# Turning the attention probabilities in squares of 32 on VectorE instead of on TensorE, in an attention + two-layer kernel in fp32

## What is computed

```python
# q, k, v: (4, 8, 576, 64), 2304 tokens of 512 values in all
mask = (rel >= 0) & (rel < 64)             # each query sees itself and 63 keys before it
attn = softmax(where(mask, q @ k.T / 8, -1e9))
x = (attn @ v)                             # as (2304, 512)
h = relu(x @ w_in);  x = (h * h) @ w_out   # first layer, 512 -> 2048 -> 512
h = x @ w_in2;  out = (h * cos(h)) @ w_out2   # second layer
```

## Time and profile before

| | us |
|---|---|
| median of 3 runs | 873.69 (873.03 to 874.81) |
| profiled execution | 873.09 |
| its span | 871.0 |
| TensorE busy in the span | 852.1 (98%), granted clock 1.0 |
| VectorE busy | 467.6 (54%) |
| ScalarE busy | 358.8 (41%) |
| GpSimd busy | 43.3 (5%) |

### The profile page before, as it was taken

One profiled execution on the slowest core, in us unless ns is written; L12 is line 12 of the kernel. 1 busy time (PEld: TensorE's weight loads), 2 busy tenths in 40 slices (PEclk: granted clock), 3 DMA queues, 4 the chain that ended last, 5 costly groups with the idle time before them and its releaser, 6 DMA issues.

```text
span 871.0 us, 13849 instructions
## 1 busy us (share of the span) xinstructions
PE 852.1 (98%) x5568; PEld 732.1 (84%) x5568; DVE 467.6 (54%) x805; ACT 358.8 (41%) x819; POOL 43.3 (5%) x51
## 2 busy tenths in 40 slices
PE   4899999999999999999999999999999999999998
PEld 4799988888888888888999888899999888888886
DVE  3776553335434453333556765666666565556554
ACT  4565443333333343323555433443444343334333
POOL 5500100000100000000000000000000000000000
PEclk9999999999999999999999999999999999999999
DMA  5645231111301130020331000300200200001001
GB/s 193 200 165 177 91 107 45 50 49 61 134 22 47 37 139 19 2 98 4 126 125 37 1 1 1 113 9 2 108 25 1 98 37 1 0 1 49 1 0 49
DMA packets 18928, 52.80 MB, mean 61 GB/s; under 512 B 2096, under 2 KB 2096, under 8 KB 17840
## 3 DMA queue, kind: packets, MB, share of 16 engines
q1 hardware_dynamic: 18864, 51.91, 17.3%
HBM read 41.42 MB, written 10.49 MB: 60 GB/s over the span
## 4 chain that ended last, share of the span: by engine, by line
PE 95%; DVE 2%; ACT 1%; DMA 1%; POOL 1%; issue 0%; SPq 0%; DVEq 0%; ACTq 0%
PE h L473 34%; PE y L515 23%; PE y L554 22%; PE st L473 11%; PE st L448 2%; PE st L417 2%; PE st L432 1%; DMA arena<-qk_duos 1%; PE y L417 1%; POOL arena L961 0%; ACT arena L625 0%; DVE arena L803 0%; DVE arena L793 0%; DVE w_out_lo L819 0%; PE h L448 0%
## 5 line engine op out<-in xcount | busy, mean ns | idle before, releaser
L824 DVE TENSOR_TENSOR act<-act 128x512 f32<-128x512 f32 (+1 forms) x80 | 51.1, 638 | 199.7 <-ACT g_hi L661 199.5
L655 ACT ACTIVATE act<-h 128x512 f32<-128x512 f32 (+1 forms) x80 | 44.4, 555 | 246.8 <-PE h L473 246.8
L832 DVE TENSOR_TENSOR g_lo<-act,g_hi 128x512 fp32r<-128x512 f32 (+1 forms) x160 | 102.5, 641 | 54.3 <-ACT g_hi L666 51.5
L515 PE MATMUL y<-g_hi,w_out_hi 128*128 128x512 f32 (+1 forms) x320 | 121.0, 378 | 1.0 <-DVE g_lo L832 1.0
L473 PE MATMUL h<-x_hi,w_in_hi 128*128 128x512 f32 (+3 forms) x488 | 120.7, 369 | 0.0
L473 PE MATMUL h<-x_hi,w_in_lo 128*128 128x512 f32 (+3 forms) x488 | 119.2, 365 | 0.0
L473 PE MATMUL h<-x_lo,w_in_hi 128*128 128x512 f32 (+3 forms) x488 | 118.8, 365 | 0.0
L515 PE MATMUL y<-g_lo,w_out_hi 128*128 128x512 f32 (+1 forms) x320 | 117.9, 369 | 0.0
L515 PE MATMUL y<-g_hi,w_out_lo 128*128 128x512 f32 (+1 forms) x320 | 117.7, 368 | 0.0
L554 PE MATMUL y<-w_out_hi,g_lo 128*128 128x512 f32 x288 | 112.7, 391 | 0.0
L554 PE MATMUL y<-w_out_lo,g_hi 128*128 128x512 f32 x288 | 112.6, 391 | 0.0
(11 more groups left out here) (81 smaller groups left out, 984.9 us busy)
## 6 DMA issues: line engine op xcount, KB each, us to landing
arena<-qk_duos SPq DMA_DIRECT2D x17, 640.0 KB, 4.4
arena<-w_in SPq DMA_DIRECT2D x32, 256.0 KB, 3.0
arena<-w_out SPq DMA_DIRECT2D x32, 256.0 KB, 2.8
arena<-v_duos SPq DMA_DIRECT2D x18, 384.0 KB, 3.5
out<-arena SPq DMA_DIRECT2D x18, 256.0 KB, 2.1
x_tiles<-x_hi SPq DMA_DIRECT2D x2, 1024.0 KB, 4.3
x_tiles<-x_lo SPq DMA_DIRECT2D x2, 1024.0 KB, 6.9
x_hi<-x_tiles SPq DMA_DIRECT2D x2, 1024.0 KB, 5.0
```

Source lines behind the costliest of these rows:

```text
L515: mm = pe.matmul(bank, w[:, f, d * P:(d + 1) * P], x[:, g % 2, c * size:(c + 1) * size], start=(s == 0 and c == 0 and n == 0 and d % per = ...
L655: nc.scalar.activation(act[:, g % 2, 0:cols1(g)], h_bank[g % 2][:, 0:cols1(g)], ACT.Relu).then_inc(relu_set, 1)
L824: nc.vector.tensor_tensor(a, a, a, ALU.mult).then_inc(sq_set, 1)
L832: nc.vector.tensor_tensor(g_lo[:, g % 2, cols], act[:, g % 2, cols], g_hi[:, g % 2, cols].bitcast(fp32), ALU.subtract).then_inc(glo_set, 1)
```

## The change

From duo 7 on (`DVE_TURNS`), TensorE's four transposes and VectorE's two spreads are gone. In their place, per duo:

- `move_squares`, on VectorE directly behind `norm` in phase 1: four transposes in squares of 32, each from 32 partitions (256 columns) to 32 other partitions. They carry the off-diagonal squares of each 64x64 square, which belong wholly to the own or wholly to the preceding block, from `prob` straight to their place in `prob_t`.
- `turn`, on VectorE behind `g_low` of phase 2: one transpose in squares of 32 over 128 partitions and 512 columns, in place in `prob`, and two `copy_predicated` of 128x512 that put the diagonal squares into `prob_t` under the two masks.

The operands of `pv` are laid out by head now. It has as many matmuls of the same size, in another order over the four quarters of the array; `v_duos` holds four pieces a duo (own and preceding, for both blocks) where it held three blocks, 512 KB instead of 384. The scores copy of a later duo waits for `prob_t_set` instead of TensorE's transposes. GpSimd clears four 32x32 squares of the mask once.

```diff
+        DVE_TURNS = duo_at[2]
+        HB = BLK // 2
...
             def pv(d):
                 pe.wait_ge(v_loaded[d % 2], 16 * (d // 2 + 1))
+                if d >= DVE_TURNS:
+
+                    pe.wait_ge(prob_t_set, 2 * d + 2)
+                    for a in range(PAIRS):
+                        for w in range(2):
+                            for b in range(2):
+                                for head in range(2):
+                                    rows, to = slice((head ^ b) * HD, ((head ^ b) + 1) * HD), slice(head * HD, (head + 1) * HD)
+                                    mm = pe.matmul(pv_cols(d)[to, b, a * BLK:(a + 1) * BLK],
+                                                   v_at[d % 2][rows, b, w, a, :], prob_t[rows, b, w, a * BLK:(a + 1) * BLK],
+                                                   start=(w == 0), stop=(w == 1),
+                                                   tile_position=((head ^ b) * HD, head * HD))
+                    mm.then_inc(pv_done, 1)
+                    return
...
-                if d is not None and phase(j, s) == 2 and g > 1:
+                if d is not None and phase(j, s) == 2 and g > 1 and d < DVE_TURNS:
                     turn(2 * d)
                     turn(2 * d + 1)
...
-                if t >= 4:
+                if t >= 2 * DVE_TURNS + 4:
+                    act_e.wait_ge(prob_t_set, t + count - 4)
+                elif t >= 4:
                     act_e.wait_ge(turned, t + count - 4)
...
+            def turn(d):
+
+                if d == DVE_TURNS:
+                    dve.wait_ge(squares_cut, 4)
+                dve.wait_ge(squares_moved, 4 * (d - DVE_TURNS + 1))
+                nc.vector.transpose(prob[:, d % 2], prob[:, d % 2]).then_inc(squares_turned, 1)
+                dve.wait_ge(squares_turned, d - DVE_TURNS + 1)
+                for w in range(2):
+                    keep = keep_t[:, w, :].rearrange("p (o c) -> p o c", o=1)
+                    nc.vector.copy_predicated(prob_t[:, :, w, :].rearrange("p b (a c) -> p b a c", c=BLK),
+                                              keep.rearrange("p (o n) c -> p o n c", o=1)
+                                              .broadcast_to([P, 2, PAIRS, BLK]).bitcast(i32),
+                                              prob[:, d % 2].rearrange("p (b a) c -> p b a c", b=2))                      .then_inc(prob_t_set, 1)
+
+            def move_squares(d):
+
+
+                dve.wait_ge(normed, 2 * d + 2 - POOL_NORMS)
+                dve.wait_ge(pv_done, d)
+                square = prob[:, d % 2].rearrange("p (b a) c -> p b a c", b=2)
+                for head in range(2):
+                    for half in range(2):
+                        of = slice(head * BLK + half * HB, head * BLK + (half + 1) * HB)
+                        keys = slice(head * BLK + (1 - half) * HB, head * BLK + (2 - half) * HB)
+                        to = prob_t[keys, :, 1 - half, :].rearrange("p b (a c) -> p b a c", c=BLK)
+                        nc.vector.transpose(to[:, :, :, half * HB:(half + 1) * HB],
+                                            square[of, :, :, (1 - half) * HB:(2 - half) * HB]).then_inc(squares_moved, 1)
...
                     if phase(j, s) == 1:
                         norm(2 * d, 2)
+                        if d >= DVE_TURNS:
+                            move_squares(d)
                     if phase(j, s) == 2 and g > 1:
-                        spread(2 * d)
-                        spread(2 * d + 1)
+                        if d < DVE_TURNS:
+                            spread(2 * d)
+                            spread(2 * d + 1)
+                        else:
+                            turn(d)
```

More of the change, by code:

```diff
@@ L4, with attention_ffn_ffn @@
 from concourse import mybir
-def attention_ffn_ffn(nc, qk_duos, v_duos, w_in1, w_out1, w_in2, w_out2, x2_dram, out):
+def attention_ffn_ffn(nc, qk_duos, v_first, v_duos, w_in1, w_out1, w_in2, w_out2, x2_dram, out):
     fp32, f32r, i32 = mybir.dt.float32, mybir.dt.float32r, mybir.dt.int32
@@ L116, in attention_ffn_ffn @@
         GROUPS = PAIRS // 2
-        Q, K, V = PAIRS * 2 * BLK, PAIRS * 3 * BLK, 3 * GROUPS * P
+        Q, K, V = PAIRS * 2 * BLK, PAIRS * 3 * BLK, 4 * PAIRS * BLK
+        V_FIRST = 3 * GROUPS * P
         DUO = Q + K + V
@@ L122, in attention_ffn_ffn @@
         qk_at = [arena[:, n * DUO:n * DUO + Q + K] for n in range(2)]
-        v_at = [arena[:, n * DUO + Q + K:(n + 1) * DUO].rearrange("p (b g h e) -> p b g h e", b=3, g=GROUPS, h=2)
-                for n in range(2)]
+        v_cols = [arena[:, n * DUO + Q + K:(n + 1) * DUO] for n in range(2)]
+        v_first_at = [v[:, 0:V_FIRST].rearrange("p (b g h e) -> p b g h e", b=3, g=GROUPS, h=2) for v in v_cols]
+        v_at = [v.rearrange("p (b w a e) -> p b w a e", b=2, w=2, a=PAIRS) for v in v_cols]
         at = 2 * DUO
@@ L176, in attention_ffn_ffn @@
         prob_t_set = sem("prob_t_set")
+        squares_cut = sem("squares_cut")
+        squares_turned = sem("squares_turned")
+        squares_moved = sem("squares_moved")
         pv_done = sem("pv_done")
@@ L251, in x_duo @@
             j, first = duo_tile(d)
-            return x_of(x, j, j % 2)[:, :, first:first + 2 * BLK].rearrange("p (g r) c -> p r g c", r=2)
+            tokens = x_of(x, j, j % 2)[:, :, first:first + 2 * BLK]
+            if d < DVE_TURNS:
+                return tokens.rearrange("p (g r) c -> p r g c", r=2)
+            return tokens.rearrange("p a (b c) -> p b a c", b=2)
         duo_at = [first // (2 * BLK) for first in START]
         FIRST_DUOS = duo_at[1]
+        DVE_TURNS = duo_at[2]
+        HB = BLK // 2
         def duo_in(j, s):
@@ L316, in load_v @@
                     sp.wait_ge(pv_done, d - 1)
-                sp.dma_start(arena[:, d % 2 * DUO + Q + K:(d % 2 + 1) * DUO], v_duos[d]).then_inc(v_loaded[d % 2], 16)
+                if d < DVE_TURNS:
+                    sp.dma_start(v_cols[d % 2][:, 0:V_FIRST], v_first[d]).then_inc(v_loaded[d % 2], 16)
+                else:
+                    sp.dma_start(v_cols[d % 2], v_duos[d - DVE_TURNS]).then_inc(v_loaded[d % 2], 16)
             def load_piece(n):
@@ L448, in pv @@
                                     mm = pe.matmul(pv_cols(d)[to, odd, (group * 2 + b) * BLK:(group * 2 + b + 1) * BLK],
-                                                   v_at[d % 2][rows, b + own, group, head, :],
+                                                   v_first_at[d % 2][rows, b + own, group, head, :],
                                                    prob_t[rows, b, 1 - own, cols:cols + BLK],
@@ L633, in x_high @@
                     act_e.wait_ge(x2_stored[j % 2], 32 * (j // 2))
-                nc.scalar.copy(x_duo(x_hi, d), pv_cols(d).rearrange("p r (g c) -> p r g c", g=GROUPS))\
+                nc.scalar.copy(x_duo(x_hi, d), pv_cols(d).rearrange("p r (n c) -> p r n c", c=x_duo(x_hi, d).shape[-1]))\
                   .then_inc(xhi_set, 1)
@@ L812, in x_low @@
                     dve.wait_ge(x2_stored[j % 2], 32 * (j // 2))
-                nc.vector.tensor_tensor(x_duo(x_lo, d), pv_cols(d).rearrange("p r (g c) -> p r g c", g=GROUPS),
+                nc.vector.tensor_tensor(x_duo(x_lo, d), pv_cols(d).rearrange("p r (n c) -> p r n c", c=x_duo(x_hi, d).shape[-1]),
                                         x_duo(x_hi, d).bitcast(fp32), ALU.subtract).then_inc(xlo_set, 1)
@@ L996, in _ @@
                 w_split(n)
-            for d in range(FRONT_DUOS, DUOS):
+            for d in range(FRONT_DUOS, DVE_TURNS + 1):
+                scale_q(d)
+            pool.wait_ge(prob_t_set, 2 * DVE_TURNS)
+            pool.wait_ge(q_scaled, DVE_TURNS)
+            for half in range(2):
+                for w in range(2):
+                    rows = slice(half * BLK + w * HB, half * BLK + (w + 1) * HB)
+                    nc.gpsimd.memset(keep_t[rows, w, (1 - w) * HB:(2 - w) * HB], 0.0).then_inc(squares_cut, 1)
+            pool.wait_ge(squares_cut, 4)
+            for d in range(DVE_TURNS + 1, DUOS):
                 scale_q(d)
@@ L1022 @@
     qk_duos = np.stack([np.concatenate([p.reshape(P, -1) for p in duo], 1) for duo in parts])
+    first = 384 // BLK // 2 + 512 // BLK // 2
     v_blocks = v_rows.reshape(-1, BLK, PAIRS // 2, 2, 2, HD).transpose(0, 3, 1, 2, 4, 5).reshape(-1, P, D // 2)
-    v_duos = np.stack([np.concatenate([v_blocks[t] for t in range(2 * d, 2 * d + 3)], 1) for d in range(DUOS)])
-    arrays = {"qk_duos": np.ascontiguousarray(qk_duos), "v_duos": np.ascontiguousarray(v_duos)}
+    v_first = np.stack([np.concatenate([v_blocks[t] for t in range(2 * d, 2 * d + 3)], 1) for d in range(first)])
+    heads = v_rows.reshape(-1, BLK, PAIRS, 2, HD).transpose(0, 3, 1, 2, 4)
+    v_duos = np.stack([np.concatenate([heads[t, order].reshape(P, -1) for t, order in (
+        (2 * d + 1, [0, 1]), (2 * d, [0, 1]), (2 * d + 2, [1, 0]), (2 * d + 1, [1, 0]))], 1)
+        for d in range(first, DUOS)])
```

(4 more changed lines are left out.)

## The result

| | before | changed |
|---|---|---|
| median | 873.57 us (4 runs) | 868.41 us (4 runs, 867.91 to 869.41) |
| profiled execution | 873.09 us | 868.59 us |
| its span | 871.0 us | 866.8 us |

The ratio is 0.994, with a 95% interval of 0.9923 to 0.9958: 5.2 us faster by the medians, 4.5 by the profiled executions, 4.2 by their spans. No run shows what makes these 0.3 us. Beside the experiments the changed kernel ran once more, 868.19 us (6 runs) against 873.15, ratio 0.9937 (0.9924 to 0.995).

A forecast was written before the change was run, and what follows sets the result against it. TensorE, busy 98% of the span, was taken to bound the kernel: 873.09 − 5.1 (transposes) + 1.1 (wait) = 869.1 us, with the median 0.6 above the profiled execution: 869.7, range 868.0 to 875.5.

The forecast's parts named there:

- the forecast case: Gain with little or no wait of TensorE, 0 to 0.28 us a duo: 868.0 to 872.0 us, chance 0.64.
- The saving: Four transposes leave TensorE's path ahead of `pv`: 0.46 us a duo, 5.1 us over eleven duos.
- pv at nothing: The new diagonal order of `pv`'s matmuls over the array's quarters changes nothing, bounds ±0.06 us a duo.
- The moves: Four VectorE transposes of 32 partitions and 256 columns behind `norm`: 0.45 us each, 0.03 between them, no overlap.
- The squaring late by 0.57: VectorE's squaring of phase 2 starts 0.57 us later because the four moves stand ahead of it.
- The big transpose: VectorE's transpose of 128x512 behind `g_low`: 0.72 us, bounds 0.43 and 1.22.
- the half-rate rival: VectorE's transposes take twice the time per column, `pv` waits 1.61 us a duo: +12.6 us, 886.3; chance 0.14.
- The copies: Two predicated copies of 128x512 completing `prob_t` on VectorE: 1.35 us together, bounds 1.29 and 1.44.
- The semaphores: Delays on VectorE of 0.10 us between `norm` and the moves, and 0.10 between big transpose and copies.
- The whole chain: VectorE from the end of `norm` at 345.64 to complete `prob_t` at 351.14, where TensorE needs it at 350.99.
- The wait: TensorE waits for `prob_t` ahead of `pv`: 0.10 us a duo, 1.1 us in all.
- The rival of the exposed chain: `pv` waits 0.3 to 0.6 us a duo for VectorE, taking the gain: +1.1 us, 874.8; chance 0.17.

The follow-up runs named there:

- kernel within one group of partitions: Changed kernel with all four moves reading and writing partitions 0 to 31, off-diagonal squares left wrong: 867.44 us, ratio to before 0.9931.
- fifth move: Changed kernel with one of the four moves done a second time, behind the others, in each of the eleven duos: 873.76 us, ratio to before 1.0.
- both remedies: Changed kernel with big transpose and copies ahead of the squaring, and GpSimd scaling queries only after the turn two duos before: 867.31 us, ratio to before 0.9922.

## Why the prediction was right

869.7 us with 868.0 to 875.5 was predicted, 868.41 came; the forecast case, a gain with little wait, is the one that happened. The result lies near the lower end of the range, and its 95% interval (866.8 to 869.9 us) reaches beyond that end. By the prediction's own terms the forecast case reaches from 867.9 to 872.4, not from 868.0 to 872.0.

- **The saving**, 0.46 us a duo, 5.1 in all: within the span it came back whole when TensorE transposed again (3.27 us from there to `pv`), while everything else stayed.
- **pv at nothing**: 1.10 us in both orders.
- **The moves**: 0.45 each and 0.03 between them were taken, 0.436 and 0.03 measured, with no overlap, as the separate partitions suggested. The kernel within one group of partitions shows why. The rule that the prediction quoted for this held; the wait of 0.15 that it set beside it didn't come, because the other links were shorter.
- **The squaring late by 0.57**: in the earlier trace rows the squaring came 1.42 us after the end of `norm`, now 344.23 − 342.32 = 1.91, so 0.49 late.
- **The big transpose** at 0.72: 0.703. This settles the half-rate rival: its moves of 0.69 would have shown in the first row. "Vector Engine (DVE) Microarchitecture Reference", section 3.8, of the Trainium skill (one element per cycle and lane) agrees: 512 columns in 0.70 us, 256 in 0.44, which is 1.04 ns a column.
- **The copies** at 1.35 for the two: 1.39, taken 0.04 too short. The only other such link is the 0.03 us between the last move and the squaring, which was taken at nothing.
- **The semaphores** at 0.10: 0.04 behind `norm` and 0.03 behind the big transpose, which made up for both.
- **The whole chain**: from the end of `norm` to the last copy it is 5.37 us where 5.50 were forecast, and the weight load of `pv` came 0.12 us after the last copy, as read from the earlier trace rows. By the prediction's own sum, which had 0.15 us with 5.50, 5.37 leaves 0.02; 0.03 was measured.
- **The wait** at 0.10 a duo, 1.1 us in all: 0.03 in nine duos and 0.30 in two, 0.87 in all. The total is right in part by luck: the sum of the links was 0.13 us too long, and 0.6 of the 0.87 comes from GpSimd's scaling in two duos, of which the prediction said nothing (only that GpSimd's memsets cost nothing).
- **Layout, transfers and the mask**: nothing. The values' 512 KB land in 3.8 us, and no row waits for them.
- **The rival of the exposed chain** was not what happened, but its warning was exact. The fifth move makes its break-even real: 0.44 us more a duo, and the gain is gone.

The median lies 1.3 us below the forecast. Sum and profiled execution are 0.5 apart (869.1 and 868.59), of which the waits explain 0.2 and the time outside the span 0.3. The other 0.8 is the step from the profiled execution to the median: 0.6 up in the three runs of before, 0.2 down in the changed kernel, both within the scatter of single runs.

## What to carry to other kernels

Moving work from the engine that bounds the kernel to an idle one pays its full time on the path, and only as long as the moment at which the result is needed is met; what counts is the chain from its first instruction to that moment, not the idle engine's busy share. Here 43% of idle time on VectorE hid a chain with no slack, in which 0.44 us more took back 5 us. In such a chain, put what the bounding engine needs first ahead of what it needs later, keep GpSimd off its neighbourhood, and let consecutive instructions of VectorE stay in one group of partitions where that is free. These three were worth 0.03 to 0.3 us a duo here; the stretches show it, the medians don't.

## What the runs showed of the hardware

- Four transposes on 32 partitions and 256 columns take 1.41 us in one group of partitions and 1.84 us when each reads and writes another group than the one before.
- A subtraction of 128x512 on VectorE took 0.98 instead of 0.69 us when GpSimd had begun its scaling during the squaring ahead of it (1.08 once, where it had begun 0.04 us before the end of the squaring). In the kernel with the fifth move GpSimd began 0.09 us before the squaring, and it was the squaring that took 1.07. This is not simply working side by side. In the kernel with both remedies GpSimd begins right behind the copies, during the squaring, in nine duos, and `g_low` is at 0.98 in all nine, free there because nobody waits for it; in the changed kernel's first duo, where GpSimd began at 122.97 during the moves, `g_low` took 0.69. Which pairing costs was not taken apart further.
- A wait of TensorE can cost more than itself. Behind waits of 3.20, 3.20 and 2.59 us its granted clock was 0.50 for 3.4 us each, from 1.0 to 1.5 us after it had begun again; behind 1.79 us this came once in eleven times; behind the waits of 0.40 to 0.79 us of the kernel with the fifth move, never.
